# Second expert layer: tokens as the stationary operand, first weights streamed in high and low parts

## The chip, the cores and the metric

The kernel runs on one core of a Trainium2 chip. The metric is the device time of one launch in microseconds (us), smaller is better. TensorE is the matrix engine, VectorE (DVE), ScalarE (ACT) and GpSimd (POOL) work on data in the on-chip memory SBUF and on TensorE's results in PSUM; SyncE (SP) issues DMAs.

## The reference

Three stages follow one another. Attention on 2 x 8 heads of 768 positions and 64 features, in which a query sees only the keys of its own cluster, gives `x` of 1536 tokens by 512 features. Then come two expert layers with 8 experts each. The second, which the change is about, is:

```
logits = x @ w_gate;  e_idx = argmax(logits);  gate_w = softmax(logits)[e_idx]
eom = 1 / (1 + exp(-(x @ w_output_gate)))
for e in range(8):                       # w1[e]: 512 x 1024, w2[e]: 1024 x 512
    h = max(x[mask] @ w1[e], 0)
    out[mask] = gate_w[mask] * eom[mask, e] * (h @ w2[e])
```

Each token goes to one expert. All is float32, and the precision asked for is more than one pass in a narrower type gives.

## The kernel before

`attention` comes first; the first expert layer's tiles begin at about 298 us of the span, the second's at 469.5 us. `experts` is built twice, for `layer` 0 and 1 (`first` is layer 0). It has a route part and a tile part. The route part computes the gate logits, ranks the tokens in each expert, and makes lists of tokens in tiles of 128 (`token_to_read`, `token_to_send`) and a table of how many tiles each expert has and where they begin. The tile part loops over experts (`tiles`, an unrolled loop over experts, in it a loop `Fori` over as many tiles as the table says); layer 1 has 10 tiles here, layer 2 has 16: experts 0 to 7 have 2, 2, 2, 2, 1, 2, 2 and 3.

Every engine runs this loop with a body of its own, and they meet only in semaphores that count tiles (`g` is the tile's number):

- TensorE (`body`, L1374): the first product in plain float32, weights stationary. For each of 8 blocks of 128 inner features it multiplies four 128x128 blocks of `W1` with the turned tokens `xT`, and the result is the inner values already turned (inner feature by token). Then `turn_x(g + 1)` (L1362) turns the next tile's tokens with four transposes and counts `x_turned`. Then it waits for `y_ready` (L1389), that is, until the previous tile's result has left PSUM bank `yp`, and makes the second product of 24 matmuls with 512 columns: high part of h by high part of W2, high by low, low by high (L1394, L1398, L1401). At the end it counts `y_done`.
- ScalarE: relu of each half of h, rounded to the high part (L1132); ahead of each expert it rounds W2 to its high part `W2H` in four pieces (L1127, two buffers).
- VectorE: low part of each half of h (L1270), copy of the turned tokens (`turn_in`, L1243), then `y_out` of this tile, which scales `yp` by the token's gate into SBUF (L1281), and `stage`, a copy of the gathered tokens `xg` into `xin` (L1237). After each expert the low part of the next W2 in four pieces (`split`, L1250).
- GpSimd (`body`, L1437): `gather_next(g + 2)` copies a column of token numbers (L1426) and issues the indirect DMA that gathers tokens (L1417). Then it waits until the previous result is written, counts `y_free` (L1440), which VectorE needs before it may overwrite `y_out`, copies the token numbers to send (L1441), waits for `y_ready` and sends the result with an indirect DMA (L1445).
- SyncE loads W2 and W1 of later experts (2 MB each, L1509) when `w2_free` and `w1_free` say that a buffer is free.

Each engine takes its instructions in the order written; a wait holds everything behind it on that engine. `warm(n)` are matmuls on zeros whose result is not used.

## Time and profile before

| | us |
|---|---|
| median of 3 runs | 689.98 (689.1 to 690.02) |
| profiled execution, its own time | 688.13 |
| its span, first to last instruction | 686.4 |
| TensorE busy in the span | 658.4 (96%) |
| VectorE, ScalarE, GpSimd busy | 409.9, 337.0, 295.2 |
| TensorE's granted clock, mean | 0.998 |

The profiled execution is 1.85 us under the median. In the rows, PE is TensorE's matmul part and PEld its load of the stationary operand, and times count from the start of the span. "POOLq" marks instructions of GpSimd's sequencer (semaphores and register arithmetic), which run ahead of the engine's own work. The line numbers are those of the kernel printed above.

### The profile page before, as it was taken

The page shows a single profiled execution, that of the slowest core. Times are in us where ns is not written, and L with a number is a line of the kernel's source. Part 1 is how long each engine was busy: PE and PEld are TensorE (multiplying, and loading weights), DVE is VectorE, ACT ScalarE, POOL GpSimd, SP SyncE. Part 2 cuts the span into 40 slices and gives each one's busy share as a digit, 9 for nine tenths or more (in the row PEclk, how much of TensorE's full clock was granted, in tenths as well). Part 3 has the DMA queues.
Part 4 walks back from the last instruction along what each step waited for, and adds up shares of the span by engine and source line. Part 5 has one row for each costly group of instructions (what it writes and reads, how often), then busy time and mean ns, then how long its engine had stood idle before and what let it go on. Part 6 is the DMA issues. An engine that isn't in the chain of part 4 may idle for free.

```text
span 686.4 us, 15791 instructions
## 1 busy us (share of the span) xinstructions
PE 658.4 (96%) x5939; PEld 564.5 (82%) x5949; DVE 409.9 (60%) x859; ACT 337.0 (49%) x507; POOL 295.2 (43%) x287
## 2 busy tenths in 40 slices
PE   8989999999999989899999999989999999999995
PEld 5569889888888876479998998547999999999894
DVE  7878888788888857755454635375245254443421
ACT  4568999999999886331334312232213213231200
POOL 4357999989999871021221322002132132122121
PEclk9999999999999999999999999999999999999999
DMA  9301231111220439748489964654545654941000
GB/s 279 94 2 47 55 86 49 47 48 48 60 82 25 143 129 334 280 131 310 160 301 349 349 241 142 233 208 130 192 160 173 248 174 172 372 176 51 19 31 32
DMA packets 45988, 105.77 MB, mean 154 GB/s; under 512 B 5459, under 2 KB 11603, under 8 KB 45936
## 3 DMA queue, kind: packets, MB, share of 16 engines
q1 hardware_dynamic: 38464, 87.65, 36.8%
q0 software_dynamic: 4544, 12.70, 5.8%
q10 hardware_dynamic: 2928, 4.72, 2.0%
q8 instruction: 34, 0.56, 0.3%
q14 instruction: 18, 0.15, 0.1%
HBM read 87.64 MB, written 13.11 MB: 147 GB/s over the span
## 4 chain that ended last, share of the span: by engine, by line
PE 53%; DVE 3%; DMA 2%; issue 1%; ACT 0%; POOL 0%; POOLq 0%; ACTq 0%; DVEq 0%
PE hT_ps_layer L1381 27%; PE y_ps_layer L1394 7%; PE y_ps_layer L1398 7%; PE y_ps_layer L1401 7%; PE x_turn_layer L1368 2%; DMA x<-x_mid 1%; PE hT_ps_layer L1310 1%; PE hT_ps_layer L1308 1%; PE x_turn_layer L1298 1%; DVE row_one_hot_layer L1210 1%; DMA x_tile_layer<-x_src,token_to_read_layer 1%; PE hT_ps_layer L1323 1%; DMA x_mid<-y_out_layer,y_token_layer 0%; PE count_ps_layer L1298 0%; PE rank_ps_layer L1298 0%
## 5 line engine op out<-in xcount | busy, mean ns | idle before, releaser
L1381 PEld LDWEIGHTS hT_ps_layer<-xT_layer,w 128*128 128x128 f32 x1664 | 189.6, 192 | 3.8 <-DVE xT_layer L1243 1.7
L1381 PE MATMUL hT_ps_layer<-xT_layer,w 128*128 128x128 f32 x1664 | 190.2, 275 | 0.8 <-issue 0.8
L438 POOL TENSOR_TENSOR probs_lo<-probs,probs_hi 128x768 f16<-128x768 f32 x89 | 146.1, 1649 | 33.0 <-ACT probs_hi L353 30.4
L1132 ACT ACTIVATE hT_hi_layer<-hT_ps_layer 128x512 fp32r<-128x512 f32 x52 | 31.1, 597 | 239.2 <-PE hT_ps_layer L1381 239.2
L565 DVE TENSOR_REDUCE max_halves<-turn 128x1 f32<-128x384 f32 x180 | 94.7, 553 | 31.8 <-PE turn L729 30.2
L1270 DVE SCALAR_TENSOR_TENSOR hT_lo_layer<-hT_ps_layer,hT_hi_layer 128x512 fp32r<-128x512 f32 x52 | 34.6, 689 | 88.0 <-ACT hT_hi_layer L1132 77.0
L345 ACT ACTIVATE probs<-scores 128x768 f32<-128x768 f32 x96 | 79.9, 832 | 11.3 <-PE scores L753 10.3
L1445 POOL DMA_INDIRECT out_dram<-y_out_layer,y_token_layer x16 | 19.7, 1234 | 147.1 <-DVE y_out_layer L1281 147.1
L353 ACT ACTIVATE probs_hi<-scores 128x768 f16<-128x768 f32 x96 | 80.2, 836 | 1.2 <-PE pv L777 0.9
L1127 ACT ACTIVATE w_hi<-w 128x1024 fp32r<-128x1024 f32 x64 | 62.4, 1047 | 26.6 <-issue 26.6
L1250 DVE TENSOR_TENSOR w_lo<-w,w_hi 128x1024 fp32r<-128x1024 f32 x64 | 74.0, 1219 | 0.0
L729 PE MATMUL turn<-kB,qB 96*128 96x384 f32 x180 | 68.6, 402 | 2.0 <-DVE max_halves L565 1.6
L1394 PE MATMUL y_ps_layer<-w_hi,hT_hi_layer 128*128 128x512 f32 x208 | 58.5, 403 | 0.0
L1401 PE MATMUL y_ps_layer<-w_hi,hT_lo_layer 128*128 128x512 f32 x208 | 56.6, 393 | 0.0
L1398 PE MATMUL y_ps_layer<-w_lo,hT_hi_layer 128*128 128x512 f32 x208 | 56.4, 393 | 0.0
L753 PE MATMUL scores<-qA,kA 128*128 128x384 f32 x192 | 54.1, 362 | 2.0 <-ACT probs_hi L353 2.0
L1445 POOL DMA_INDIRECT x_mid<-y_out_layer,y_token_layer x10 | 15.9, 1592 | 81.3 <-DVE y_out_layer L1278 81.3
L1281 DVE TENSOR_SCALAR y_out_layer<-y_ps_layer,slot_gate_layer 128x512 f32<-128x512 f32 x16 | 12.0, 752 | 63.5 <-PE y_ps_layer L1401 63.5
L753 PE MATMUL scores<-qB,kB 99*128 99x384 f32 x192 | 49.6, 339 | 0.0
L1398 PEld LDWEIGHTS y_ps_layer<-w_lo,hT_hi_layer 128*128 128x128 f32 x208 | 39.1, 188 | 9.1
L1401 PEld LDWEIGHTS y_ps_layer<-w_hi,hT_lo_layer 128*128 128x128 f32 x208 | 38.9, 188 | 9.0 <-DVE hT_lo_layer L1270 0.4
L776 PE MATMUL pv<-v_hi_and_one,probs_hi 128*128 128x65 f16 x576 | 46.2, 194 | 0.0
(227 smaller groups left out, 1087.5 us busy)
## 6 DMA issues: line engine op xcount, KB each, us to landing
w<-in_moe_w_dram SPq DMA_DIRECT2D x32, 2048.0 KB, 11.2
w<-in_v_dram ACTq DMA_DIRECT2D x4, 768.0 KB, 7.1
qk_raw<-in_q_dram SPq DMA_DIRECT2D x16, 192.0 KB, 3.2
qk_raw<-in_k_dram SPq DMA_DIRECT2D x16, 192.0 KB, 3.5
qB<-qA SPq DMA_DIRECT2D x16, 192.0 KB, 2.7
kB<-kA SPq DMA_DIRECT2D x16, 192.0 KB, 3.1
x_src<-x SPq DMA_DIRECT2D x2, 1536.0 KB, 17.0
x_mid<-x SPq DMA_DIRECT2D x2, 1536.0 KB, 18.3
```

Source lines behind the costliest of these rows:

```text
L345: nc.scalar.activation(probs[slot][:].rearrange("p (n c) -> p n c", n=2), sc[kt % 2][:, :, 0:HALF], ACT.Exp, scale=SCALE).then_inc(probs_r ...
L353: nc.scalar.activation(p_hi[slot][:].rearrange("p (n c) -> p n c", n=2), sc[kt % 2][:, :, 0:HALF], ACT.Exp, scale=SCALE).then_inc(probs_re ...
L438: nc.gpsimd.tensor_tensor(p_lo[slot][:], probs[slot][:], p_hi[slot][:], ALU.subtract).then_inc(p_lo_pool, 1)
L565: nc.vector.tensor_reduce(mh[:, u // 2, u % 2:u % 2 + 1], turn[b][:, 0:HALF], AX.X, ALU.max).then_inc(turn_free[b], 1)
L729: nc.tensor.matmul(turn[b][:, 0:HALF], QB[r][0:ROWS_MASK, t * P:(t + 1) * P], KB[r][0:ROWS_MASK, n * HALF:(n + 1) * HALF], start=True, sto ...
L753: m = nc.tensor.matmul(sc[kt % 2][:, n, 0:HALF], lhs[:, kt * P:(kt + 1) * P], rhs[:, n * HALF:(n + 1) * HALF], start=(part == 0), stop=(pa ...
L1127: nc.scalar.activation(W2H[par][:, c, :], W2[par][:, c, :], ACT.Copy).then_inc(w2_hi, 1)
L1250: nc.vector.tensor_tensor(W2L[:, c, :], W2[par][:, c, :], W2H[par][:, c, :].bitcast(F32), ALU.subtract).then_inc(w2_lo, 1)
L1381: t = nc.tensor.matmul(hp[n][:, i * P:(i + 1) * P], W1[par][:, c, f * P:(f + 1) * P], xT[:, c, :], start=(c == 0), stop=(c == CD - 1))
L1394: nc.tensor.matmul(yp[:], hH[:, f, :], W2H[par][:, f, :], start=(f == 0), stop=False)
L1398: nc.tensor.matmul(yp[:], hH[:, f, :], W2L[:, f, :], start=False, stop=False)
L1401: t = nc.tensor.matmul(yp[:], hL[:, f, :], W2H[par][:, f, :], start=False, stop=(f == CF - 1))
```

## The change

In the second layer only (in the first the body stays):

- The first product has the tokens as the stationary operand and W1 as the moving one, 512 columns at a time. Tokens and W1 are split into a high and a low part; three of the four products are made, 24 matmuls per tile. Its result is h with tokens on the partitions, so after relu (`hR`) TensorE turns it in eight transposes (`turn_h`), and ScalarE and VectorE take the high and low parts from the turned copy.
- `W1H` lies where the second buffer of `W2H` was, `W1L` where `W2L` was; `W2L` gets new room. So there is one `W2H`, and ScalarE waits for `y_done` of the last tile of the expert before it writes it. W1 of the next expert is split after the last tile of an expert, four pieces on ScalarE and four on VectorE. For expert 0 this is done at the end of layer 1.
- No staging: tokens are gathered straight into `xin`, so the gather for tile g + 2 waits for `turn_x(g + 1)`.
- The result of a tile leaves PSUM one tile later: `y_out(g)` takes the result of tile g - 1, and one more step follows after the loop. Column 0 of the gates and of the send list is filled so that step 0 sends nothing.

```diff
+    W1H, W1L = (a[:].rearrange("p c n -> p (c n)").rearrange("p (c f) -> p c f", f=F) for a in (W2H[1], W2L))
...
+    AHEAD = 0 if first else 1
+    send_all = sb("token_to_send", [P, AHEAD + NT_COLS], U32)
+    gate_all = sb("slot_gate", [P, AHEAD + NT_COLS], F32)
+    send_tok, gate_of = send_all[:, AHEAD:AHEAD + NT_COLS], gate_all[:, AHEAD:AHEAD + NT_COLS]
+    if first:
+        ring = sb("x_tiles", [P, RING, DM], F32)
+        xg = sb("x_gathered", [P, DM], F32)
+        xin = sb("x_tile", [P, DM], F32)
+        xT = sb("xT", [P, CD, P], F32)
+        hH = sb("hT_hi", [P, CF, P], F32R)
+        hL = sb("hT_lo", [P, CF, P], F32R)
+        yout = sb("y_out", [P, DM], F32)
+    else:
+        parts = [a[:].rearrange("p a b -> p (a b)") for a in x_both]
+        hH, hL = (a[:, 0:F].rearrange("p (c n) -> p c n", n=P) for a in parts)
+        xTH, xTL = (a[:, F:F + DM] for a in parts)
+        place = Xt[:].rearrange("p t b r -> p (t b r)")
+        hR = place[:, 0:F]
+        xin, yout = (place[:, F + n * DM:F + (n + 1) * DM] for n in range(2))
+        W2H = W2H[0:1] * 2
+        W2L = sb("w2_rest", [P, CF, DM], F32R)
...
+    gate_ps = (lp[:, 0:3 * NT_COLS] if first else tp[1][:, P:P + 3 * NT_COLS]).rearrange("p (v t) -> p v t", t=NT_COLS)
+    hT = [lp, cp]
...
+            def split(e, pair, par, base):
 
                 act.wait_ge(w2_ready[par], 16 * (pair + 1 + layer * E // 2))
+                if not first:
+                    act.wait_ge(y_done, base + 1)
...
+            def x_to_hi(g):
+                act.wait_ge(x_turned, g + 1)
+                nc.scalar.activation(xTH, tp[0][:], ACT.Copy).then_inc(x_hi, 1)
+            def w1_part(par, i):
+                n, c = slice(i // 2 * F // 2, (i // 2 + 1) * F // 2), slice(i % 2 * CD // 2, (i % 2 + 1) * CD // 2)
+                nc.scalar.activation(W1H[:, c, n], W1[par][:, c, n], ACT.Copy).then_inc(w1_hi, 1)
+            def h_to_hi(g, n):
+                act.wait_ge(h_turned[n], g + 1)
+                nc.scalar.activation(hH[:, n * (CF // 2):(n + 1) * (CF // 2), :].rearrange("p c n -> p (c n)"), hT[n][:],
+                                     ACT.Copy).then_inc(h_hi, 1)
+            def body_turned(g, pair, par):
+                act.wait_ge(h_done[0], g + 1)
+                nc.scalar.activation(hR[:, 0:F // 2], hp[0][:], ACT.Relu).then_inc(h_kept[0], 1)
+                h_to_hi(g, 0)
+                act.wait_ge(h_done[1], g + 1)
+                nc.scalar.activation(hR[:, F // 2:F], hp[1][:], ACT.Relu).then_inc(h_kept[1], 1)
+                x_to_hi(g + 1)
+                h_to_hi(g, 1)
+            def w1_split(e, pair, par):
+                if isinstance(e, int) and e == E - 1:
+                    return
+                act.wait_ge(w1_ready[1 - par], 16 * (pair + par + 1 + E // 2))
+                for i in range(W1_STEPS):
+                    w1_part(1 - par, i)
+            if first:
+                tiles(act, body, split, after)
+                act.wait_ge(w1_ready[0], 16 * (1 + E // 2))
+                act.wait_ge(weights_over, 1)
+                for i in range(W1_STEPS - 1):
+                    w1_part(0, i)
+            else:
+                x_to_hi(0)
+                tiles(act, body_turned, split, w1_split)
...
+            def w1_piece(i):
+                return slice(i % 2 * CD // 2, (i % 2 + 1) * CD // 2), slice(i // 2 * F // 2, (i // 2 + 1) * F // 2)
+            def w1_rest(e, par):
+                for i in range(W1_STEPS):
+                    c, n = w1_piece(i)
+                    if first and i == W1_STEPS - 1:
+                        nc.vector.tensor_copy(W1H[:, c, n], W1[par][:, c, n]).then_inc(w1_hi, 1)
+                    dve.wait_ge(w1_hi, W1_STEPS * e + i + 1)
+                    nc.vector.tensor_tensor(W1L[:, c, n], W1[par][:, c, n], W1H[:, c, n].bitcast(F32), ALU.subtract).then_inc(w1_lo, 1)
+                dve.wait_ge(w1_lo, W1_STEPS * e + W1_STEPS)
+                dve.sem_inc(w1_free, 1)
...
+                nc.vector.memset(gate_all[:, 0:1], 0.0).then_inc(none_sent, 1)
+                nc.vector.memset(send_all[:, 0:1], NO_TOKEN).then_inc(none_sent, 1)
...
+            def x_to_lo(g):
+                dve.wait_ge(x_hi, g + 1)
+                nc.vector.tensor_tensor(xTL, tp[0][:], xTH.bitcast(F32), ALU.subtract).then_inc(x_lo, 1)
...
+                dve.wait_ge(none_sent, 2)
+                dve.wait_ge(gates_turned, 1)
+                nc.vector.tensor_reduce(gate_of, gate_ps.rearrange("p v t -> p t v"), AX.X, ALU.add).then_inc(gates_out, 1)
+                x_to_lo(0)
...
+            def h_to_lo(g, n):
+                dve.wait_ge(h_hi, 2 * g + n + 1)
+                half = slice(n * (CF // 2), (n + 1) * (CF // 2))
+                nc.vector.tensor_tensor(hL[:, half, :].rearrange("p c n -> p (c n)"), hT[n][:],
+                                        hH[:, half, :].rearrange("p c n -> p (c n)").bitcast(F32), ALU.subtract).then_inc(h_lo, 1)
+            if not first:
+                dve.wait_ge(gates_out, 1)
+            def y_out(g):
+                dve.wait_ge(y_free, g + 1)
+                dve.wait_ge(y_done, g + 1)
+                nc.vector.tensor_scalar(yout, yp[:], col(gate_all, g), None, ALU.mult).then_inc(y_ready, 1)
+            def body_turned(g, pair, par):
+                y_out(g)
+                h_to_lo(g, 0)
+                x_to_lo(g + 1)
+                h_to_lo(g, 1)
 
             def after(e, pair, par):
                 if not (isinstance(e, int) and e == E - 1):
+                    if not first:
+                        w1_rest(e + 1, 1 - par)
                     split(e + 1, None, 1 - par)
-            tiles(dve, body, after=after)
+            tiles(dve, body if first else body_turned, after=after)
+            if first:
+                w1_rest(0, 0)
+            else:
+                y_out(steps(dve))
...
+            def turn_h(g, n):
+                pe.wait_ge(h_kept[n], g + 1)
+                for i in range(CF // 2):
+                    f = n * (CF // 2) + i
+                    t = nc.tensor.transpose(hT[n][:, i * P:(i + 1) * P], hR[:, f * P:(f + 1) * P], ident[:])
+                t.then_inc(h_turned[n], 1)
+            def body_turned(g, pair, par):
+                e = 2 * pair + par
+                pe.wait_ge(x_lo, g + 1)
+                for n in range(2):
+                    at = slice(n * F // 2, (n + 1) * F // 2)
+                    for c in range(CD):
+                        if c % 2 == 0:
+                            pe.wait_ge(w1_hi, W1_STEPS * e + 2 * n + c // 2 + 1)
+                        nc.tensor.matmul(hp[n][:], xTH[:, c * P:(c + 1) * P], W1H[:, c, at], start=(c == 0), stop=False)
+                        nc.tensor.matmul(hp[n][:], xTL[:, c * P:(c + 1) * P], W1H[:, c, at], start=False, stop=False)
+                    if n == 1:
+                        turn_h(g, 0)
+                    for c in range(CD):
+                        if c % 2 == 0:
+                            pe.wait_ge(w1_lo, W1_STEPS * e + 2 * n + c // 2 + 1)
+                        t = nc.tensor.matmul(hp[n][:], xTH[:, c * P:(c + 1) * P], W1L[:, c, at], start=False, stop=(c == CD - 1))
+                    t.then_inc(h_done[n], 1)
+                turn_x(g + 1)
+                pe.wait_ge(y_ready, g + 1)
+                for n in range(2):
+                    half = range(n * (CF // 2), (n + 1) * (CF // 2))
+                    pe.wait_ge(h_hi, 2 * g + n + 1)
+                    for f in half:
+                        nc.tensor.matmul(yp[:], hH[:, f, :], W2H[par][:, f, :], start=(f == 0), stop=False)
+                    if n == 0:
+                        turn_h(g, 1)
+                    pe.wait_ge(w2_lo, W2_STEPS * e + 2 * n + 2)
+                    for f in half:
+                        nc.tensor.matmul(yp[:], hH[:, f, :], W2L[:, f, :], start=False, stop=False)
+                    pe.wait_ge(h_lo, 2 * g + n + 1)
+                    for f in half:
+                        t = nc.tensor.matmul(yp[:], hL[:, f, :], W2H[par][:, f, :], start=False, stop=(f == CF - 1))
+                t.then_inc(y_done, 1)
+            tiles(pe, body if first else body_turned)
...
-            pool.sem_inc(y_ready, 1)
+            pool.sem_inc(y_ready if first else y_done, 1)
...
+                gather(xin, read_tok[:, 0:1], x_in)
+                pool.wait_ge(x_turned, 1)
+                gather(xin, read_tok[:, 1:2], x_in)
+                pool.wait_ge(none_sent, 2)
+                pool.wait_ge(to_send, 1)
...
+            def body_turned(g, pair, par):
+                pool.wait_ge(x_turned, g + 2)
+                nc.gpsimd.tensor_copy(gid[:], col(read_tok, g + 2)).then_inc(gid_ready, 1)
+                pool.wait_ge(gid_ready, g + 1)
+                pool.sem_inc(may_gather, 1)
+                gather(xin, gid[:, 0:1], x_in)
+                send(g)
+            def send(g):
+                pool.wait_ge(y_sent, 16 * g + 16)
+                pool.sem_inc(y_free, 1)
+                nc.gpsimd.tensor_copy(yid[:], col(send_all, g)).then_inc(yid_ready, 1)
+                pool.wait_ge(yid_ready, g + 1)
+                pool.wait_ge(y_ready, g + 1)
+                pool.sem_inc(may_send, 1)
+                nc.gpsimd.indirect_dma_start(out=result[:, :], out_offset=bass.IndirectOffsetOnAxis(ap=yid[:, 0:1], axis=0),
+                                             in_=yout, in_offset=None, bounds_check=n_tok - 1, oob_is_err=False).then_inc(y_sent, 16)
+            tiles(pool, body if first else body_turned)
+            n_tiles = steps(pool)
+            if not first:
+                send(n_tiles)
+            pool.wait_ge(y_sent, 16 * (n_tiles + AHEAD) + 16)
```

## Rows read from the trace of the kernel before

**Rows 1.** The page: busy time of TensorE, its share of the span, instructions.
```profile
PE 658.4 (96%) x5939; PEld 564.5 (82%) x5949; DVE 409.9 (60%) x859; ACT 337.0 (49%) x507; POOL 295.2 (43%) x287
```

**Rows 2.** Busy time by stage; columns are named in the first row.
```profile
core 0: us, PE busy (x) PEld busy (x) DVE busy (x) ACT busy (x) POOL busy (x), PEclk, DMA share, GB/s
...
469.00:679.00 210.00, 209.76 (x1474) 193.37 (x1472) 84.29 (x112) 46.42 (x60) 46.57 (x63) 1.00 0.44 155
```

**Rows 3.** Chain of waits in one tile of layer 2: start us, us, what.
```profile
548.25 7.14 PE hT_ps_layer L1381 x64
555.39 0.44 PE x_turn_layer L1368 x4
555.83 0.92 PE y_ps_layer L1394 x4
...
561.33 0.78 PE hT_ps_layer L1381 x7
```

**Rows 4.** Groups by line in layer 2: busy us, mean ns, idle before.
```profile
L1250 DVE TENSOR_TENSOR w_lo<-w,w_hi 128x1024 fp32r<-128x1024 f32 x32 | 37.0, 1219 | 0.0
...
L1127 ACT ACTIVATE w_hi<-w 128x1024 fp32r<-128x1024 f32 x28 | 27.3, 1047 | 6.5 <-issue 6.5
...
L1132 ACT ACTIVATE hT_hi_layer<-hT_ps_layer 128x512 fp32r<-128x512 f32 x32 | 19.1, 597 | 154.8 <-PE hT_ps_layer L1381 154.8
```

**Rows 5.** Timeline, end of one tile: start us, us, engine, what.
```profile
542.15 0.60 PE L1368 MATMUL x_turn_layer<-ident,x_tile_layer 128*128 128x128 f32 x4
...
542.50 1.16 PE L1394 MATMUL y_ps_layer<-w_hi,hT_hi_layer 128*128 128x512 f32 x4
...
547.17 1.08 PE L1401 MATMUL y_ps_layer<-w_hi,hT_lo_layer 128*128 128x512 f32 x4
...
548.46 0.75 DVE L1281 TENSOR_SCALAR y_out_layer<-y_ps_layer,slot_gate_layer 128x512 f32<-128x512 f32 x1 [4.20 <-PE y_ps_layer L1401]
```

**Rows 6.** GpSimd lines L1426 (549 to 562 us), L1428 and L1440 (469 to 472.8): ns, first and last start.
```profile
L1426 POOLq FUSED_REGOPS  x1: 46/46/46, 551.4 to 551.4; - x1
L1426 POOL COPY gather_token_layer<-token_to_read_layer x1: 260/260/260, 551.6 to 551.6; 128x1 uint32 x1
...
L1428 POOLq EVENT_SEMAPHORE  x1: 17/17/17, 471.0 to 471.0; - x1
...
L1440 POOLq EVENT_SEMAPHORE  x1: 17/17/17, 471.7 to 471.7; - x1
```

**Rows 7.** Gathers of tokens, GpSimd line L1417, in layer 2.
```profile
DMA to landing us min/median/max: 3.4/3.7/7.0
```

**Rows 8.** Timeline of ScalarE in layer 2: first and last of seven groups of W2.
```profile
491.50 3.91 ACT L1127 ACTIVATE w_hi<-w 128x1024 fp32r<-128x1024 f32 x4 [0.88 <-issue]
...
635.20 3.90 ACT L1127 ACTIVATE w_hi<-w 128x1024 fp32r<-128x1024 f32 x4 [0.69 <-issue]
```

**Rows 9.** Timeline of TensorE at the start, and after its longest later wait.
```profile
1.33 6.50 PE L665 MATMUL pv<-blank 128*128 128x512 bf16 x16 [1.33 <-DVE blank L485]
7.66 0.38 PE L673 MATMUL cluster_logits_ps<-ident,centroids_hi_lo 128*128 128x128 f32 x2
7.88 1.03 PE L665 MATMUL pv<-blank 128*128 128x512 bf16 x4
...
43.80 0.50 PE L739 MATMUL turn<-ident_b,max_parts 128*3 128x128 bf16 x6 [1.59 <-DVE max_parts L589]
44.22 0.62 PE L753 MATMUL scores<-qA,kA 128*128 128x384 f32 x2
```

**Rows 10.** Timeline between the layers: start us, us, engine, what.
```profile
430.12 7.29 PE L1323 MATMUL hT_ps_layer<-blank 128*128 128x512 bf16 x33
...
431.35 0.42 DVE L1239 COPY x_tiles_layer<-x_gathered_layer 128x512 f32 x1
...
434.67 1.52 ACTq L1085 DMA_DIRECT2D x<-x_mid  x3
...
437.70 0.20 DVE L1145 CAST gate_weights_hi_lo_layer<-wg 128x64 fp32r<-128x64 f32 x1 [5.93 <-PEq L1087]
```

115 lines of the change are left out of this document (58 added, 57 removed).

## Prediction

> **What bounds the kernel now.** I read the page's busy times first, then the busy times by stage, the chain of waits, the groups of layer 2 by line, and at last the timeline around one tile. TensorE is busy for 96% of the span [rows 1], and in layer 2 for 209.76 of 210 us at the full clock, while VectorE, ScalarE and GpSimd have 84, 46 and 47 us [rows 2]. The chain of a tile has nothing but TensorE in it: 7.14 us first product, 0.44 turning the next tokens, 24 second matmuls at 0.92 per four, and the next tile begins 13.08 us after the last (561.33 - 548.25) [rows 3]. So each TensorE instruction taken out of a tile is worth its full time, sixteen times, and every wait put into TensorE's order costs its full time too. The other engines have room, but only where they do not have to answer TensorE.
>
> **TensorE's work per tile.** The new first product is 24 matmuls of 512 columns, the form of the second product, which goes at 0.92 / 4 = 0.229 us each [rows 3]: 5.50 us. Eight more 128x128 transposes at 0.44 / 4 = 0.11 us [rows 3]: 0.87 us. The tile's work is 5.50 + 0.87 + 0.44 + 5.50 = 12.31 us against 13.08, a gain of 0.77, and 16 x 0.77 = 12.3 us. Loads of the stationary operand stay hidden as in the second product, which has the same form. Bounds: none of this work is new in kind.
> A transpose in the rows lasts 0.60 us for four with their overlap [rows 5], and they start 0.11 us apart. The Trainium skill (TensorE: Matmul & The Clock Gate, Part 4: PE-mode transpose) gives about 275 ns for a 128x128 transpose in one kernel. Counted at that price in full, the eight would cost 2.2 us and the tile would be 0.6 us longer than before, 9 us over sixteen; the chain speaks against it, since four of them take it 0.44 us. I give this 0.01, at 724.7 + 16 x 1.33 = 746.
>
> **The wait that the later result adds.** This is the term that decides. Before the second product of tile g TensorE waits for `y_ready` g + 1. That count now comes from `y_out(g)`, which VectorE runs only after `y_free` g + 1. GpSimd gives that in `send(g)`, behind its wait for `x_turned` g + 2, the copy of token numbers and the gather. And `x_turned` g + 2 is `turn_x(g + 1)`, which TensorE does right before it waits. So in every tile, TensorE turns the tokens, stops, and goes on only after a round trip over GpSimd and VectorE, although the result of tile g - 1 has long been done. In the kernel before GpSimd's `y_free` hung on nothing of the same tile's TensorE work, and the gap there is zero [rows 3]. Step by step:
> - The last transpose ends at 542.75, 0.25 us after the second product had begun at 542.50 [rows 5]: 0.25.
> - GpSimd wakes and starts the copy: 0.2 from its register step at 551.4 to the copy at 551.6 [rows 6], and 0.1 for the signal: 0.30.
> - The copy, 0.26 and 0.04 to the next step at 551.9 or so: 0.30 [rows 6].
> - From the step after the copy (L1428) to `y_free` (L1440): 471.7 - 471.0 = 0.70 [rows 6]. That is a tile where the previous write had long landed, as it will have here. The gather's issue lies between them in the program, but `y_free` is the sequencer's and did not wait for it.
> - VectorE wakes and passes a second wait: TensorE's end at 547.17 + 1.08 = 548.25 to the scaling at 548.46 is 0.21 [rows 5]; with the second wait 0.30.
> - The scaling: 0.75 [rows 5]. Back to TensorE: 0.10, my value, with 0.21 as the nearest row's bound.
> The sum is 2.70 us. Lower bound 2.35 (no second wait, no signal time at GpSimd, 0.05 back); upper bound 3.9, if `y_free` does have to wait for a gather's issue of 1.1 us or so. Nothing can hide it: the waits are in a ring with TensorE in it. Queued behind `y_out(g)` on VectorE are the low parts of h and the next tokens, each 0.7 us. TensorE wants the first of these 8 matmuls and 4 transposes (2.3 us) after it goes on; they are in time. Queued behind GpSimd's wait is the send, which nobody wants for another tile.
> Net per tile 2.70 - 0.77 = 1.93 us; 16 tiles: +30.9 us. Bounds: 16 x (2.35 - 0.77) = 25.3 and 16 x (3.9 - 0.77) = 50.
>
> **Change of expert.** There are seven (28 pieces of W2 in groups of four) [rows 4, 8]. In a tile's own time (0 where it starts, wait included it is 15.0 long) ScalarE rounds the second half of the turned h at 10.6 to 11.2, then four pieces of W1 in 3.9 us [rows 8], to 15.2. VectorE follows, four at 1.14 (1.219 with overlap, rows 4), to 17.0, 2 us into the next tile. TensorE takes the pieces in the order in which they are made and needs the low ones of the first half at 1.8 and of the second at 5.1: no wait. ScalarE then writes W2's high part, after `y_done`: from 0.3 to 4.2 us of the new tile. Behind this stands its relu of the first half, 0.60 [rows 4], to 4.8 and with signals 5.0, and TensorE wants to turn that half after 20 matmuls, at 4.58. A wait of 0.2 to 0.7, I take 0.5: 3.5 us over seven. VectorE's low parts of W2 end about 6.7 us in, before `y_free` comes at 7.9, so they are covered by the wait above; without it they would be just in time. Bounds: nothing, and 5.1 us each (ScalarE's four pieces and one of VectorE, 3.9 + 1.2, wholly in TensorE's way), 36 in all. I stay near the lower end because each engine's order can be read off. Room for W1 and W2 comes free earlier than before relative to its use, so I cost the loads at nothing.
>
> **Staging, ends, route.** Without `stage` and `turn_in` VectorE is freed from 1.1 us per tile that was not in the chain: nothing. A gather is now issued one tile ahead of its use, over 13 us, and lands in 3.6 us, at most 7.0 [rows 7]: nothing. Between the layers, ScalarE's three pieces of W1 lie at 430.5 to 433.4, before its own DMAs at 434.67. VectorE's four subtractions and a copy start when the last result is out, about 431.8 [rows 10], and take some 5.6 us to 437.4, while the warm matmuls end at 437.41 (430.12 + 7.29) [rows 10]: level, up to 0.4 late. Two small memsets stand in the route's chain: +0.2. Tokens of tile 0 need a high and a low part instead of one copy, and the warm matmuls cover most: +0.1. So +0.3, between 0 and 1.2. At the very end the last result takes the same way as before.
>
> **Sum.** +30.9 + 3.5 + 0.3 = +34.7 us: 688.13 + 34.7 = 722.8 for an execution like the profiled one, whose span of 686.4 leaves 1.7 outside. The median shown is 1.85 above that execution, so I give 724.7.
>
> **Rivals.**
> - *The wait is as forecast and the clock falls in it.* TensorE now stands idle for 2.7 us in every tile. At the start of the kernel, sixteen matmuls took 7.66 - 1.33 = 6.3 us where they later take 0.217 each (7.88 and 1.03 for four), which is the lower level, 1.2 GHz, and a loss of 2.9 us [rows 9]. For it: no idle time as long as this is in the trace after the start. Against it: after 1.59 us idle at 43.80 the clock was still granted in full and two matmuls of 384 columns took 0.62 us [rows 9]. With half of the loss, 1.45 us a tile, the time would be 724.7 + 23 = 748, with all 771. The Trainium skill (TensorE: Matmul & The Clock Gate, Part 1: The HAM clock gate) says that an idle stretch takes the clock back to 1.2 GHz; no row of this kernel shows a fall.
> - *The change of expert is exposed.* If TensorE has to wait for half of the W1 pieces, 2.5 us more each: 724.7 + 7 x 2.5 = 742. For it: one buffer for each high and low part now. Against: the order of the pieces follows their use.
> - *The wait is half as long.* If sequencers answer faster than their rows, 1.35 us: 16 x 0.58 + 3.5 + 0.3 = +13.1, 703.
> - *Faster.* If `y_free` g + 1 were out before the first product and turn of tile g end (GpSimd's wait for `x_turned` g + 2 satisfied earlier than I read), the result of tile g - 1 would leave PSUM under the first product. Then only TensorE's work counts: -12.3 + 3.5 + 0.3 = -8.5, 681.5. It decides at a wait of 0.77 - 3.8 / 16 = 0.53 us per tile, below which the kernel is faster. For it stands that layer 2's chain is TensorE only [rows 3]; against it, the counts in the code.
>
> **How the numbers follow.** Chances: forecast 0.70, clock 0.10, change of expert 0.07, half wait 0.05, faster 0.06, 0.01 for dear transposes and 0.01 that it all cancels. The forecast's own range is 718 (25.3 + 2) to 745 (every step late). The range of 711 to 748 holds it, the change of expert and half of the clock's case, and leaves out 703, 681.5 and the slower clock: near 2 in 10. A change of 0.2%, 1.4 us, is what can be told from none. Slower: 0.93; faster 0.06; the same 0.01.
>
> **What would show it.** Right: in layer 2, an idle time of 2.35 to 3.9 us ahead of L1394's successor in each of sixteen tiles, ended by `y_out`; `y_out` waiting for GpSimd and no more for TensorE; the first product at 5.5 us; the tile at about 15 us. Seven short waits of the turning of h for ScalarE. Wrong: TensorE's busy share in layer 2 stays near 100%, or the granted clock drops there, or the first product's matmuls come further apart than 0.229 us.

## The result, and the profile after

The changed kernel takes 737.4 us (median of 4 runs, 736.9 to 737.71) against 689.54 (median of 4, 688.8 to 690.02) for the one before: ratio 1.0694, 95% interval 1.0676 to 1.0713, 47.9 us slower. Forecast were 724.7, range 711 to 748. The profiled execution took 737.57 us for a span of 735.9.

Busy times on the page of the changed kernel, the line that answers to [rows 1]:

```profile
PE 669.5 (91%) x5436; PEld 548.0 (74%) x5437; DVE 442.4 (60%) x878; ACT 393.4 (53%) x587; POOL 289.2 (39%) x289
```

Busy time by stage (columns in the first row). The last row is layer 2 and answers to [rows 2]; the two in the middle lie in the attention, more than 350 us before anything that the change touches:

```profile
core 0: us, PE busy (x) PEld busy (x) DVE busy (x) ACT busy (x) POOL busy (x), PEclk, DMA share, GB/s
...
45.00:50.00 5.00, 3.90 (x28) 3.59 (x28) 2.09 (x5) 2.89 (x5) 1.65 (x1) 0.53 0.00 0
50.00:60.00 10.00, 9.80 (x98) 8.65 (x96) 7.23 (x16) 7.22 (x13) 4.49 (x4) 0.89 0.16 40
...
470.00:720.00 250.00, 214.94 (x959) 172.06 (x959) 110.14 (x123) 102.11 (x139) 37.99 (x61) 0.93 0.37 130
```

TensorE had been busy for 209.76 of 210 us at clock 1.00 in this layer. Now it is busy for 215 of 250, at 0.93: it waits, and it is slowed. What it waits for stands in the waits (engine and line waited for: us in total, times, longest):

```profile
POOL gather_token_layer L1625 <- PE x_turn_layer L1498: 181.8, 16, 12.6
DVE x L1396 <- POOLq L1634: 108.4, 16, 12.3
...
PE y_ps_layer L1562 <- DVE x L1396: 36.5, 16, 2.8
```

These three lines are the ring that the prediction read from the code: GpSimd waits for TensorE's turn, VectorE's `y_out` for GpSimd's `y_free`, TensorE for `y_out`, in each of sixteen tiles. The chain of waits gives its steps. Here is one tile that is not the first of its expert, from the last work before the turn (it answers to [rows 3]; start us, us, what; the "q" rows are sequencers):

```profile
494.92 0.45 PE x_turn_layer L1498 x4
495.39 0.04 POOLq L1625
495.43 0.07 issue
...
495.53 0.17 POOL gather_token_layer L1625
...
495.84 0.51 issue
496.35 0.04 POOLq L1633
...
496.59 0.76 DVE x L1396
497.35 0.12 issue
497.47 1.19 PE y_ps_layer L1562 x4
```

From the end of the turn at 495.37 to 497.47 TensorE stands still for 2.10 us; the copy of token numbers is over at 495.70, and `y_free` follows at 496.35. In the same view this tile's first product began at 489.03, with 16 pieces of 0.23 and two groups of four at 0.91 and 0.92 before the turn.

The same view of the first tile of an expert:

```profile
539.30 3.42 DVE w_rest_layer L1342 x3
...
543.37 0.32 DVEq L1094
...
544.10 0.30 DVEq L1095
...
545.09 0.76 DVE x L1396
545.85 0.12 issue
545.98 1.19 PE y_ps_layer L1562 x4
547.16 0.84 PE count_ps_layer L1535 x4
548.01 1.71 PE y_ps_layer L1567 x4
549.72 1.33 PE y_ps_layer L1570 x4
551.04 0.91 PE y_ps_layer L1562 x4
```

Two things are new in it. VectorE ends its last piece of W2 at 542.72 (539.30 + 3.42) and begins `y_out` only at 545.09: its sequencer leaves one loop, reads the count and the base of the next expert from the table (L1094, L1095) and enters the next. And after the wait four matmuls take 1.71 us where they take 0.91 at the full clock: TensorE is back at 1.2 GHz for a while.

Laid beside the profiled execution of before, the 49.4 us (737.57 - 688.13) come from five places:

| place | us | how it is read |
|---|---|---|
| the ring, net of the saved work | 25.1 | 16 x (14.65 - 13.08), a tile without clock loss, first product to first product |
| clock after the wait | 15.6 | 10 of 16 tiles, 1.56 each |
| first tiles of an expert | 4.4 | their wait is up to 0.65 longer; the relu is late in seven, which costs TensorE 0.17 each |
| between the layers | 1.8 | first product of layer 2 at 474.00 and not 469.50, less the next line |
| attention | 2.7 | clock 0.53 and 0.89 after an idle time of 1.60 us that every kernel here has; not of the change (below) |

### The profile page after: what moved, and what is told of

The parts are those of the page before. It is cut to its first block, busy times and chain, and to the rows that moved or that the text cites. A ratio compares the mean times of both kernels' runs of the same rounds, so it can differ in the third digit from the quotient of the medians.

```text
span 735.9 us, 14926 instructions
## 1 busy us (share of the span) xinstructions
PE 669.5 (91%) x5436; PEld 548.0 (74%) x5437; DVE 442.4 (60%) x878; ACT 393.4 (53%) x587; POOL 289.2 (39%) x289
## 4 chain that ended last, share of the span: by engine, by line
PE 43%; DVE 10%; issue 4%; DMA 2%; DVEq 1%; ACT 1%; POOL 0%; ACTq 0%; POOLq 0%
PE hT_ps_layer L1511 10%; PE y_ps_layer L1562 5%; PE y_ps_layer L1567 4%; DVE w_rest_layer L1342 4%; PE y_ps_layer L1570 4%; PE hT_ps_layer L1554 2%; PE hT_ps_layer L1548 2%; PE hT_ps_layer L1547 2%; PE y_ps_layer L1522 2%; PE y_ps_layer L1526 2%; PE y_ps_layer L1529 2%; DVE x L1396 2%; DVE w_lo L1233 2%; PE count_ps_layer L1535 1%; PE x_turn_layer L1498 1%
## 5 line engine op out<-in xcount | busy, mean ns | idle before, releaser
L1511 PEld LDWEIGHTS hT_ps_layer<-xT_layer,w 128*128 128x128 f32 x640 | 72.9, 192 | 1.8 <-DVE xT_layer L1335 1.0
L1511 PE MATMUL hT_ps_layer<-xT_layer,w 128*128 128x128 f32 x640 | 73.2, 275 | 0.5 <-issue 0.5
L1562 PE MATMUL y_ps_layer<-w_hi,xT_hi_layer 128*128 128x512 f32 x128 | 38.9, 428 | 36.5 <-DVE x L1396 36.5
L1562 PEld LDWEIGHTS y_ps_layer<-w_hi,xT_hi_layer 128*128 128x128 f32 x128 | 24.1, 198 | 44.7 <-issue 40.3
L1168 ACT ACTIVATE hT_hi_layer<-hT_ps_layer 128x512 fp32r<-128x512 f32 x20 | 11.9, 597 | 84.4 <-PE hT_ps_layer L1511 84.4
L1547 PE MATMUL hT_ps_layer<-w_hi,xT_hi_layer 128*128 128x512 f32 x128 | 49.9, 390 | 0.4 <-DVE xT_lo_layer L1349 0.4
L1548 PE MATMUL hT_ps_layer<-w_hi,xT_lo_layer 128*128 128x512 f32 x128 | 49.8, 389 | 0.0
L778 PE MATMUL pv<-v_lo,probs_hi 128*128 128x64 f16 x576 | 46.2, 195 | 0.0
L777 PEld LDWEIGHTS pv<-v_hi_and_one,probs_hi 128*128 128x128 f16 x576 | 38.1, 99 | 8.3 <-issue 3.2
L1567 PE MATMUL y_ps_layer<-w_rest_layer,xT_hi_layer 128*128 128x512 f32 x128 | 43.7, 471 | 0.0
```

Source lines behind the costliest of these rows:

```text
L777: nc.tensor.matmul(pv_o[:, t, :], p, v_hi[r][:, kt, 0:D + 1], start=False, stop=False, skip_group_check=True)
L1511: t = nc.tensor.matmul(hp[n][:, i * P:(i + 1) * P], W1[par][:, c, f * P:(f + 1) * P], xT[:, c, :], start=(c == 0), stop=(c == CD - 1))
L1547: nc.tensor.matmul(hp[n][:], xTH[:, c * P:(c + 1) * P], W1H[:, c, at], start=(c == 0), stop=False)
L1548: nc.tensor.matmul(hp[n][:], xTL[:, c * P:(c + 1) * P], W1H[:, c, at], start=False, stop=False)
L1562: nc.tensor.matmul(yp[:], hH[:, f, :], W2H[par][:, f, :], start=(f == 0), stop=False)
L1567: nc.tensor.matmul(yp[:], hH[:, f, :], W2L[:, f, :], start=False, stop=False)
```

## The experiments

In all of them the attention and layer 1 are untouched, but for the end of layer 1 in e7. `may_write(g)` below is the pair `wait_ge(y_sent, 16 * g + 16)`, `sem_inc(y_free, 1)`, taken out of `send`.

**e1_free_first: the ring opened.**

```diff
 def body_turned(g, pair, par):
+    may_write(g)
     pool.wait_ge(x_turned, g + 2)
```

> The changed kernel, with one thing moved: in layer 2 GpSimd waits for the last write and counts y_free before it waits for x_turned, so that VectorE may overwrite the result tile while TensorE is still in the first product. Theory (the wait is a ring over GpSimd): the nine tiles that are not the first of an expert lose their wait of 2.3 us and the clock stays up after them; in the seven first tiles of an expert y_out still stands on VectorE behind the low parts of W2 and two reads of the tile table, which in the changed kernel's trace end only some 2.7 us after the turn of the next tokens, so a wait of about that length stays there. 689.5 - 12 (TensorE's work) + 8 x 2.7 + 3 (other waits at a change of expert) + 2 (between the layers) = 704, up to 6 more if the clock falls in the waits that are left. Rival (the wait has another releaser: the result's own product or VectorE's order in every tile): no change, 735 to 738. Rival (the ring is the whole loss and a change of expert costs nothing): 682.

Measured: 712.3 us (711.79 to 718.78), ratio 1.0317 [1.0298, 1.0335]: 25 us less than the changed kernel, for two lines moved. The tiles that are not the first of an expert take 12.25 us, with no wait, which is TensorE's work as forecast (12.31). The time is 2 us over the 710 that were allowed for. What stays are eight waits at first tiles:

```profile
PE y_ps_layer L1562 <- DVE x L1396: 21.7, 8, 3.2
```

VectorE in such a tile (start us, us, engine, line, instruction, idle before):

```profile
499.68 4.63 DVE L1233 TENSOR_TENSOR w_lo<-w,w_hi 128x1024 fp32r<-128x1024 f32 x4 [0.26 <-ACT w_hi L1180]
504.45 4.63 DVE L1342 TENSOR_TENSOR w_rest_layer<-w,w_hi 128x1024 fp32r<-128x1024 f32 x4
511.01 0.75 DVE L1396 TENSOR_SCALAR x<-y_ps_layer,slot_gate_layer 128x512 f32<-128x512 f32 x1 [1.93 <-issue]
```

Eight subtractions in a row, then 1.93 us of sequencer work, then the result that TensorE wants. The mechanism of the ring is confirmed; the change of expert costs more than was allowed, since its waits are longer and bring a fall of the clock with them. (The execution shown took 718.78 us at a mean clock of 0.968; the four others, 711.79 to 712.88, have 0.978 to 0.981.)

**e2_free_after_turn: which part of the ring costs what.**

```diff
     pool.wait_ge(x_turned, g + 2)
+    may_write(g)
     nc.gpsimd.tensor_copy(gid[:], col(read_tok, g + 2)).then_inc(gid_ready, 1)
```

> The changed kernel, with y_free counted after the wait for x_turned but before the copy of token numbers and the gather. Theory (the ring, step by step): the ring keeps TensorE's turn, GpSimd's wake-up, VectorE's scaling, and loses the copy (0.2 us) and the step from L1628 to y_free (0.7 us), so the ordinary tiles' wait is 0.9 us shorter, 1.4 instead of 2.3; the first tiles of an expert change little, since VectorE is late there by itself. 737.4 - 9 x 0.9 = 729 if the clock still falls in as many tiles, 714 if no shorter wait makes it fall. Rival (the time from the turn to the second product is VectorE's or TensorE's): 737.

Measured: 726.13 us (725.9 to 729.03), ratio 1.0533 [1.0503, 1.0562]. The wait of an ordinary tile falls by 0.95 of its 2.10 us, so the copy and the steps up to the gather are some 45% of it, and the handovers between engines and VectorE's 0.75 the rest:

```profile
555.87 0.60 PE L1498 MATMUL x_turn_layer<-ident,x 128*128 128x128 f32 x4
557.62 1.18 PE L1562 MATMUL y_ps_layer<-w_hi,xT_hi_layer 128*128 128x512 f32 x4 [1.15 <-DVE x L1396]
```

After these eight waits of 1.15 us no tile shows a lower clock. The eight first tiles still wait 2.2 to 3.2 us, and each is slowed after it.

**e3_warm_in_wait: the clock by itself.** Ten matmuls of zeros keep TensorE busy while it would wait.

```diff
     turn_x(g + 1)
+    warm(10, bank=tp[1])
     pe.wait_ge(y_ready, g + 1)
```

> The changed kernel, with ten matmuls of 512 columns on zeros into a free PSUM bank between TensorE's turn of the next tokens and its wait for y_ready: 10 x 0.216 = 2.2 us, inside the wait of 2.3. Theory (TensorE's clock falls because it stands idle): the ten tiles in which the second product's first half took 1.6 us more run at full clock, 737.4 - 16 = 722, the granted clock of layer 2 is 1.00, and the wait itself stays. Rival (those tiles are slow for another reason, reading or writing memory beside VectorE): 737, and the matmuls stay far apart. Rival (the added matmuls hold TensorE): over 740.

Measured: 723.5 us (722.74 to 724.23), ratio 1.0486 [1.0465, 1.0508], 13.9 us less than the changed kernel, with nothing else moved: ordinary tiles take 14.62 us as before, and the granted clock of the layer is back:

```profile
474.00:700.00 226.00, 220.17 (x1037) 166.91 (x1051) 108.83 (x120) 98.74 (x134) 36.85 (x60) 1.00 0.40 143
```

So the fall of the clock is a cost of its own of 14 to 16 us, and TensorE's idleness is its cause.

**e4_result_at_end: the ring opened, `y_out` moved behind the low parts.** `y_free` comes first on GpSimd, as in e1. On VectorE `y_out(g + 1)` ends the body; on TensorE the high part of W1's last quarter comes after the low parts of its first half.

```diff
 def body_turned(g, pair, par):
-    y_out(g)
     h_to_lo(g, 0)
     x_to_lo(g + 1)
     h_to_lo(g, 1)
+    y_out(g + 1)
```

> The new first product without its waits: y_free counted first as in e1_free_first; y_out at the end of VectorE's body, for the tile just done, ahead of the low parts of the next W1 and W2; and TensorE's first product ordered high parts of half 0, high parts of half 1 by the first two blocks, low parts of half 0, rest, so that the low pieces of W1 are wanted later and ScalarE's relu has time behind the high parts of W2. Theory: a tile takes TensorE's 12.3 us, a change of expert 0.3 more, and 2 us are lost between the layers: 689.5 - 12 + 2 + 2 = 681.5. Rival (two-part tokens and weights in the first product cost more than the stationary weights whatever the waits): over 689.5. Rival (VectorE is the bound at a change of expert): 7 x 1.5 more, 692.

Measured: 726.09 us (724.35 to 727.17), ratio 1.052 [1.0493, 1.0547]. A miss by 45 us. VectorE's pieces of both weights now stand behind `y_out`, which waits for the end of the tile, and the low part of h comes behind them (timeline):

```profile
499.35 0.75 DVE L1401 TENSOR_SCALAR x<-y_ps_layer,slot_gate_layer 128x512 f32<-128x512 f32 x1 [3.68 <-POOLq L1645]
500.02 4.62 DVE L1233 TENSOR_TENSOR w_lo<-w,w_hi 128x1024 fp32r<-128x1024 f32 x4
504.79 4.63 DVE L1342 TENSOR_TENSOR w_rest_layer<-w,w_hi 128x1024 fp32r<-128x1024 f32 x4 [0.15 <-DVE w_lo L1233]
511.18 0.69 DVE L1391 TENSOR_TENSOR xT_lo_layer<-rank_ps_layer,xT_hi_layer 128x512 fp32r<-128x512 f32 x1 [1.75 <-issue]
```

TensorE in the list of waits of the same kernel:

```profile
PE y_ps_layer L1581 <- DVE xT_lo_layer L1391: 25.3, 7, 4.0
```

The wait has only changed what it is for. At a change of expert VectorE has 9.3 us of pieces in one block, and whatever stands behind the block is late.

**e5_pool_half: half of the W2 pieces to GpSimd.** `y_free` for the next tile at the end of GpSimd's body, and pieces 2 and 3 of W2's low part on GpSimd ahead of the expert's first tile:

```diff
+def w2_half(e, pair, par, base):
+    for i in range(W2_STEPS // 2, W2_STEPS):
+        pool.wait_ge(w2_hi, W2_STEPS * e + i + 1)
+        nc.gpsimd.tensor_tensor(W2L[:, c, :], W2[par][:, c, :], W2H[par]..., ALU.subtract).then_inc(w2_lo_pool, 1)
```

> The changed kernel with two things taken off the way of y_out: GpSimd counts y_free for the next tile as soon as this tile's result is written (before it waits for x_turned), and the low parts of the last two pieces of each W2 are made by GpSimd, with w2_free counted there, so that VectorE's queue at a change of expert is two subtractions (2.3 us) shorter and has no wait for them ahead of its two reads of the tile table. Theory (after the ring, VectorE's queue at a change of expert is the only large loss, about 3 us of wait each and the clock's fall behind some): ordinary tiles 12.25 us, first tiles of an expert under 13.2, 689.8 - 12 + 2 + 8 x 0.7 = 685. Rival (GpSimd's subtractions slow VectorE's, or are late for the second half of the second product): first tiles stay over 15 us, 705 to 712. Rival (the loss at a change of expert is ScalarE's wait for y_done): the same.

Measured: 696.11 us (695.82 to 699.4), ratio 1.0111 [1.0075, 1.0147], 11 us over the forecast. First tiles are down to 12.4 us. Two things changed on VectorE at once, and no run parts them: it has two pieces less, and it no longer waits for its own last piece before it leaves the loop, so that `y_out` begins right behind that piece and not 1.9 us later. (Leaving that wait out alone, with all four pieces on VectorE, was not tried.) But the tiles after the first ones wait for `y_out`, 9.9 us in six waits. The reason is in GpSimd's timeline:

```profile
499.74 5.70 POOL L1642 TENSOR_TENSOR w_rest_layer<-w,w_hi 128x1024 fp32r<-128x1024 f32 x2 [5.04 <-ACT w_hi L1164]
...
507.24 1.06 POOL L1589 DMA_INDIRECT x<-x_mid,gather_token_layer  x1 [1.23 <-issue]
...
509.43 1.04 POOL L1653 DMA_INDIRECT out_dram<-x,y_token_layer  x1 [0.93 <-POOL y_token_layer L1649]
...
517.03 0.18 POOL L1627 COPY gather_token_layer<-token_to_read_layer 128x1 uint32 x1 [6.55 <-DMA out_dram<-x,y_token_layer]
```

The first piece takes 3.33 us, since VectorE's last one lies over its start, and the second 2.40; the send comes behind the gather at 509.43, and `y_free` has to wait for it to land.

**e6_pool_half_order**: e5 with e4's order on TensorE.

> As e5_pool_half, and TensorE's first product in the order high parts of half 0, high parts of the first two blocks of half 1, low parts of half 0, the rest, so that half 0 of h is complete 0.9 us later but ScalarE has longer for W2's high part before the turn of half 0 is wanted. Theory: the wait of 0.3 to 0.4 us before the first turn of h in the first tile of an expert shrinks, 2 us less than e5_pool_half, 683. Rival (that wait is already under another one): the same as e5_pool_half within 1 us.

Measured: 697.5 us (695.71 to 699.55), ratio 1.0113 [1.0076, 1.0149]: the same as e5, as its rival had it. First tiles take 12.43 us, as in e5: the order of the pieces is worth nothing that shows.

**e7_no_low_at_end: who holds the send between the layers.** Leaves out VectorE's four subtractions for W1's low part of expert 0, at the end of layer 1.

```diff
+if first:
+    dve.sem_inc(w1_lo, 1)
+    continue
 nc.vector.tensor_tensor(W1L[:, c, n], ..., ALU.subtract).then_inc(w1_lo, 1)
```

> The changed kernel, leaving out VectorE's four subtractions for the low part of W1 of expert 0 at the end of layer 1 (expert 0's first product then uses what lay in that room). Read from the profile alone: in the changed kernel GpSimd's last issue of layer 1 took 1.84 us instead of 1.03. Theory (VectorE's subtractions slow GpSimd's issue): 1.0 to 1.1 us here, and the reload of x is issued 0.8 us earlier after the last result than in the changed kernel (4.35 instead of 5.16 us after y_out's start). Rival (the issue is slow for another reason, as the DMA queue): it stays at 1.8.

Measured in one profiled execution (737.35 us; in a single one, 1 us cannot be told from the clock's chance), so only its send of layer 1's last tile counts. In the timeline of the kernel before:

```profile
431.97 1.03 POOL L1445 DMA_INDIRECT x_mid<-y_out_layer,y_token_layer  x1 [8.81 <-DVE y_out_layer L1278]
```

In that of the changed kernel:

```profile
434.73 1.84 POOL L1620 DMA_INDIRECT x_mid<-y_out_layer,y_token_layer  x1 [8.81 <-DVE y_out_layer L1379]
```

And in this one's:

```profile
433.24 1.03 POOL L1623 DMA_INDIRECT x_mid<-y_out_layer,y_token_layer  x1 [8.81 <-DVE y_out_layer L1382]
```

The issue takes 1.03 us, 1.84 beside VectorE's subtractions, and 1.03 again without them. Beyond these three, the other ten executions that were profiled have the subtractions, and 1.83 or 1.84. Everything of layer 2 waits for this write: the tokens' reload starts 5.16 us after the last `y_out` begins in the changed kernel and 4.35 us in this one.

**e8_send_first: the send ahead of the gather.**

```diff
 def body_turned(g, pair, par):
+    send(g)
     pool.wait_ge(x_turned, g + 2)
     ...
     gather(xin, gid[:, 0:1], x_in)
-    send(g)
+    may_write(g + 1)
```

> As e5_pool_half, with GpSimd's body in the order: send this step's result, then wait for x_turned and gather, then wait for the write and count y_free for the next step. In e5_pool_half the first tile of an expert takes 12.4 us, but in six of the second ones y_out waits up to 2.5 us for y_free, since GpSimd's two subtractions of 2.8 us, the gather and only then the send stand in one queue. Theory (y_free comes late only through that order): the write is under way 2 us earlier and lands under the gather's issue, no tile waits for y_out, all tiles 12.3 to 12.5: 16 x 12.37 = 198 instead of 222 in e5_pool_half's trace, less the clock's falls with it, 696 - 20 + 1 = 683 (against 689.4 for the kernel before: 0.99). Rival (the write itself lands late, or GpSimd's subtractions are the bound): some second tiles keep a wait, 688 to 695.

Measured: 689.71 us (687.06 to 691.64, 12 runs), ratio 0.9994 [0.9979, 1.0009]. No wait for `y_out` is left anywhere. In its place, five tiles that follow the first tile of an expert wait for their tokens, 6.7 us in all, since the gather is now last in GpSimd's queue. This is the rival's time, 688 to 695. The late gather alone does not do it: behind the last two changes of expert the queue is the same and no tile waits, and there the loads of weights are over (a DMA share of 0.10 from 620 to 650 us in e9, of 0.45 to 0.73 between 500 and 620).

**e9_send_first_order**: e8 with TensorE's order of e4.

> As e8_send_first with TensorE's first product in the order of e6_pool_half_order. Theory: no wait is left for the order to take away (e6_pool_half_order was the same as e5_pool_half): within 1 us of e8_send_first. Rival (first tiles of an expert have 0.15 us of waits each): 1 to 2 us less.

Measured: 687.65 us (685.98 to 690.82, 12 runs), ratio 0.9972 [0.9957, 0.9986]: the first that is faster than the kernel before, by 1.9 us. It is also 2 us under e8, as its rival said, but the order is not shown to be the cause. From layer 2's first product to that of its last tile e8 takes 194.51 us (473.67 to 668.18) and e9 194.54 (471.44 to 665.98), with first tiles of 12.41 and 12.40. The two executions differ before layer 2, where the kernels are alike: in the first 60 us e8's clock is 0.94 and e9's 1.00, and e8's layer 1 begins 2.5 us later. Against the kernel before, the same stretch of layer 2 is 1.8 us shorter (196.30 there) and the last tile with the end 0.8, while the start of layer 2 is 1.9 later; so of the 1.9 us by medians the pair of profiled executions shows 0.6. TensorE's wait in the list of waits:

```profile
PE x_turn_layer L1500 <- DMA x<-x_mid,gather_token_layer: 6.7, 5, 2.0
```

**e10_one_piece: three pieces on VectorE, one on GpSimd.** e9, with `w2_half` making piece 3 alone.

> As e9_send_first_order, but GpSimd makes only the last of the four low pieces of each W2 and VectorE three. In e9_send_first_order five second tiles of an expert wait 0.9 to 2.2 us for the gather of the next tokens, which GpSimd issues only after its two pieces and the send, and which then lands in up to 7.3 us beside the weights' loads. Theory (the gather is late through GpSimd's pieces): it is issued 2.8 us earlier and the waits go, while y_out of the first tile comes 1.1 us later, at about 6.1 us of a tile in which TensorE wants it at 6.4: all tiles 12.3 to 12.5, 687.65 - 7.5 = 680. Rival (the weights' loads hold the gather whenever it is issued): some waits stay, 685 to 688. Rival (VectorE is now late for y_out): first tiles over 12.8, 687 or more.

Measured: 696.13 us (694.2 to 698.93), ratio 1.0098 [1.0074, 1.0123]. A miss, by 16 us; its rival (VectorE late for `y_out`) had the time. The gather is in time again, but VectorE is not. Its third piece of W2, the piece of GpSimd at the same time, and `y_out` (timeline):

```profile
502.48 3.41 DVE L1343 TENSOR_TENSOR w_rest_layer<-w,w_hi 128x1024 fp32r<-128x1024 f32 x1
502.40 2.40 POOL L1652 TENSOR_TENSOR w_rest_layer<-w,w_hi 128x1024 fp32r<-128x1024 f32 x1 [7.71 <-ACT w_hi L1164]
505.82 0.73 DVE L1398 TENSOR_SCALAR x<-y_ps_layer,slot_gate_layer 128x512 f32<-128x512 f32 x1
```

TensorE waits for it in seven tiles:

```profile
PE y_ps_layer L1572 <- DVE x L1398: 12.7, 7, 1.8
```

`y_out` is 1.8 us late in every first tile but that of expert 0. It is not the length of the queue that does it. A piece takes VectorE 1.22 us; this one takes 3.41 in each of the seven, since GpSimd's begins 0.08 us ahead of it, and it ends 1.08 us after GpSimd's. The 2.19 us above a piece's length are more than TensorE's wait of 1.82. So two and two is the best split that was tried; three and one with the two pieces kept apart in time was not tried.

**e11_numbers_early: e9 with the token numbers copied at the end of the body.**

```diff
     gather(xin, gid[:, 0:1], x_in)
     may_write(g + 1)
+    nc.gpsimd.tensor_copy(yid[:], col(send_all, g + 1)).then_inc(yid_ready, 1)
+    pool.wait_ge(x_in, 16 * (g + 3))
+    nc.gpsimd.tensor_copy(gid[:], col(read_tok, g + 3)).then_inc(gid_ready, 1)
```

> e9_send_first_order with one thing changed on GpSimd: the numbers of the next send and of the next gather are copied at the end of a tile's body, as soon as the write and the gather before them have landed, and no more right before the issue. In the trace of e9 the body that follows two pieces of W2 low issues its send at 506.99, 1.3 us after the copy of its numbers at 505.52, and its gather at 509.12, 0.9 us after the copy at 508.04; the tile after it then waits for the landing (6.7 us over 5 tiles, longest 2.0). Theory: these two waits between a copy and its issue are what makes the gather late. Without them the send goes out at about 505.4 and the gather at 506.5, 2.6 us earlier, more than the longest wait: the 6.7 us go, and 687.65 becomes 681 (679.5 to 683), the granted clock in layer 2 at 1.00 or close to it. Rival A: the landing beside the loads of weights is what is late (up to 7.3 us where others take 4), and an earlier issue meets the same loads: some of the waits stay, 684 to 687. Rival B: the copy for the gather now waits for the landing of the gather before, the next send stands behind it, and y_out of the next tile comes late: waits for VectorE's y_out of 1 us or more in the tiles after a change of expert, 687 to 692.

Measured: 686.21 us (685.26 to 688.12), ratio 0.9936 [0.9916, 0.9956], 3.7 us faster than the kernel before and the best of this study. It is only part of the expected gain, in the range of rival A. From layer 2's first product to that of its last tile it takes 192.4 us, where e9 takes 194.5. TensorE's waits in layer 2:

```profile
PE x_turn_layer L1500 <- DMA x<-x_mid,gather_token_layer: 4.4, 4, 2.0
PE y_ps_layer L1577 <- POOL w_rest_layer L1655: 1.6, 1, 1.6
```

VectorE's timeline behind a change of expert:

```profile
496.19 4.63 DVE L1234 TENSOR_TENSOR w_lo<-w,w_hi 128x1024 fp32r<-128x1024 f32 x4 [0.25 <-ACT w_hi L1181]
```

GpSimd's at the same time:

```profile
498.64 1.08 POOL L1649 COPY y_token_layer<-token_to_send_layer 128x1 uint32 x1 [2.37 <-DMA out_dram<-x,y_token_layer]
499.70 1.16 POOL L1644 COPY gather_token_layer<-token_to_read_layer 128x1 uint32 x1
502.21 5.73 POOL L1655 TENSOR_TENSOR w_rest_layer<-w,w_hi 128x1024 fp32r<-128x1024 f32 x2 [1.35 <-ACT w_hi L1164]
509.46 1.05 POOL L1665 DMA_INDIRECT out_dram<-x,y_token_layer  x1 [1.52 <-issue]
510.82 1.03 POOL L1597 DMA_INDIRECT x<-x_mid,gather_token_layer  x1 [0.31 <-issue]
```

The tile begins at 498.97 here and at 496.24 in e9. The pieces start 3.24 us into it in both. But the send follows them after 1.52 us although its numbers are long there, so it gains only 0.26 us (10.49 into the tile, 10.75 in e9), and the gather 1.03 (11.85, 12.88). What stands between piece and send is not the copy, as the theory had it, but GpSimd's own sequencer on its way into the loop. Rival A has the rest: gathers beside loads of weights land in up to 8.2 us. Rival B did not come as it was written, since no tile waits for `y_out`; but what it feared came once. In the tile at 586.56 GpSimd's copy waits for a gather's landing until 594.57, the pieces behind it start 9.6 us into the tile (7.1 in e9), and TensorE waits 1.6 us for them, the second line above.

## Why the prediction was right, and where it was off

*Direction and mechanism.* Right. e1 takes the ring away and with it 25.1 us of 47.9; e2 takes away 0.95 us of it per tile and the time follows. (That the table has 25.1 us for the ring too is chance: there it is sixteen tiles net of the saved work, in e1 the waits of eight tiles and the clock behind them.)

*The number.* 12.7 us under the time, and in the range by some luck. In the profiled pair, where the forecast is 14.8 us under, the terms are off by -5.8 (the ring), +15.6 (the clock), +0.9 (change of expert), +1.5 (between the layers) and +2.7 (attention): the ring was costed too high and hid a part of what the clock took, and the range held the measured time since it had room for half of the clock's case.

*TensorE's work per tile, 12.31.* Right: 12.25 in e1, 12.24 to 12.40 in e9. Four transposes take 0.44 to 0.45 us in the chain. One record of a transpose does last 0.27 us, so the figure of the Trainium skill (TensorE: Matmul & The Clock Gate, Part 4: PE-mode transpose) agrees as the length of one; as the price of one in this stream, where they start 0.11 us apart, it does not hold.

*The wait, 2.70.* It came to 2.35 (2.10 in the chain and the 0.25 by which the last transpose overlaps), which is the lower bound as stated. That bound was added up wrongly: what it leaves out (0.09, 0.10 and 0.05) takes 2.70 to 2.46, so the wait came out a little under it. The steps over GpSimd and to VectorE were each 0.06 to 0.14 us shorter than costed, the one back to TensorE 0.02 longer. GpSimd woke in 0.16 (forecast 0.30), the copy took 0.22 with its tail (0.30), `y_free` came 0.60 later (0.70), and the step to VectorE took 0.24 (0.30). It was read rightly that `y_free` does not wait for the gather's issue. In the sum the term was 30.9 and measured 25.1.

*The clock.* This is the step that failed. It was a rival at 0.10 and half of it came true: 10 of 16 tiles, 13.9 us by e3. The reason against it was one row, 1.59 us of idleness after which the clock held [rows 9]. That row was weak evidence in two ways. It is shorter than the wait that was forecast; and the changed kernel's own execution has the same gap, 1.60 us at 43.76, with the clock at 0.53 behind it. What the runs bear out, over TensorE's waits of more than 0.5 us in layer 2 in the profiled executions of the changed kernel and all experiments (a fall counts when it begins within 1.5 us of the wait's end):

| TensorE idle, us | waits | followed by a fall of the clock |
|---|---|---|
| 0.56 to 1.69 | 29 | 0 |
| 1.81 to 2.02 | 15 | 5 |
| 2.08 to 2.21 | 27 | 15 |
| 2.38 to 3.96 | 31 | 30 |

The changed kernel has eleven waits in the third row, five with a fall, and five in the last, all with one. The Trainium skill (same page, Part 1: The HAM clock gate) has an idle stretch take the clock back to 1.2 GHz; these traces agree, and show between 1.8 and 2.2 us gaps that do and gaps that do not.

*Change of expert, 3.5.* It measured 4.4 behind the ring, near enough, but mostly for another reason. ScalarE's relu is late in each of seven, but what waits 0.37 us for it is the load of the stationary operand; the next turn of tokens ends only 0.17 us later for it (6.66 and 6.49 us into the tile), 1.2 us in all where 3.5 were forecast. Not seen was the end of VectorE's loop, 2.4 us from its last piece to `y_out`: the pieces were covered by the ring's wait as forecast, the result behind them was not, and made the wait longer by 0.4 to 0.65 us in five first tiles (2.6 in all). With the ring gone the pieces of W1 end 1.8 us into the tile and those of W2 6.6 (e1: 504.31 and 509.08, the tile begins at 502.46), which is what was worked out (2 and 6.7). "Just in time" was still wrong by 2.8 us: the last piece ends with the turn, and behind it come 1.93 for the sequencer, 0.75 for the scaling and the way back. A fall of the clock follows six of e1's eight such waits.

*Between the layers, +0.3.* 1.8. The issue of the last write takes 0.8 us longer beside the subtractions, which had been costed at nothing (e7). The tokens' reload takes 8.96 us from its issue to TensorE's first turn, where it took 8.23; it takes 9.02 in e7, so this is not of the subtractions, and its cause is open. The two-part tokens add 0.2.

*Faster, 0.06.* The rival named the condition rightly, `y_free` before the first product ends, and a wait under 0.53 us. But 681.5 needed more than that: e1 meets the condition in the ordinary tiles and is still 22 us slower, and it took GpSimd as a second maker of weights and a loop of VectorE without a wait at its end (e5), its queue in another order (e8, e9) and earlier copies (e11) to come to 686.2. Whether 681.5 can be had is open: waits for tokens of 4.4 us stay, and a second buffer for them was not tried.

*Attention, 2.7 of the profiled pair.* Layer 1's first tile begins at 300.65 and not 297.92. Not of the change: the stretch of 1.59 or 1.60 us idle near 44 us is there in all thirteen profiled executions, and a fall of the clock follows it in nine, in five of them before the next gap there, of 1.1 us at about 46 us. The executions of the kernel before, e2, e5 and e9 have no fall and begin layer 1 at 297.8 to 298.2 us, those of the changed kernel and the rest at 299.0 to 300.65.

## What to carry to other kernels

Where a kernel is bound by one engine, look for rings: a count that this engine waits for and that, by way of two other queues, hangs on something it has done in the same step. One such ring costs its whole length each time, and freeing a buffer one line earlier in a helper's queue can be worth more than the work that a new algorithm saves (25.1 us here, against 12.3). When the ring is gone the next limit is the burst, here weights made at a change of expert: spread it over engines by what stands behind it in each queue, and count the loop's end and the table reads as work.
